# Local attention: one 32x128 matmul for both heads' values of a query tile, and x written by two additions of 64 partitions

## The reference

```python
def _attn_ref(q, k, v):                   # 4 batches, 8 heads, 576 positions, head size 64
    # coarse part: full attention on means of 4 positions (144 x 144), repeated 4 times
    out_up = np.repeat(sm_attn(q_d, k_d, v_d), factor, axis=2)
    # local part: only keys nearer than 4 positions
    mask = np.abs(pos[:, None] - pos[None, :]) < factor
    ... attn = softmax(scale * q @ k^T where mask) ...
    return out_up + attn @ v

a = x @ w1; b = x @ w2                    # first MLP:  2304 x 512 -> 1024
x = ((a * b) @ w3) @ w_out                #             -> 512
h = max(x @ u1, x @ u2, x @ u3)           # second MLP: 512 -> 768
out = h @ u_out                           #             -> 512
```

## Time and profile before

| | before |
|---|---|
| median of 3 runs | 726.11 us (725.23 to 726.60) |
| the profiled execution, its own time | 725.54 us |
| its span, first to last instruction | 723.8 us |
| PE busy | 713.2 us (99%), 6560 matmuls |
| PE weight loads busy | 595.1 us (82%) |
| DVE, ACT, POOL busy | 219.8, 193.0, 210.9 us (30%, 27%, 29%) |
| granted TensorE clock | full in every slice of the span |
| L385 matmuls (local values) | 1536, 18.4 us |
| L571 (x_out) | 16, 12.1 us, 757 ns each |

### The profile page before, as it was taken

One profiled execution on the slowest core, in us unless ns is written; L12 is line 12 of the kernel. 1 busy time (PEld: TensorE's weight loads), 2 busy tenths in 40 slices (PEclk: granted clock), 3 DMA queues, 4 the chain that ended last, 5 costly groups with the idle time before them and its releaser, 6 DMA issues.

```text
span 723.8 us, 14645 instructions
## 1 busy us (share of the span) xinstructions
PE 713.2 (99%) x6560; PEld 595.1 (82%) x6560; DVE 219.8 (30%) x392; ACT 193.0 (27%) x417; POOL 210.9 (29%) x186
## 2 busy tenths in 40 slices
PE   6999999999999999999999999999999999999998
PEld 4778788888888888888888998888888888888898
DVE  3464554414453345411100455111111111111111
ACT  5465423322332233312221533111120112111110
POOL 5799423303232223321220231130122114011210
PEclk9999999999999999999999999999999999999999
DMA  9874122202221121122000320000001000000100
GB/s 321 264 233 142 53 74 74 74 24 75 74 75 54 54 92 58 40 80 81 1 1 0 117 73 1 1 35 24 1 0 60 1 0 25 34 1 1 43 16 29
DMA packets 18590, 43.57 MB, mean 60 GB/s; under 512 B 2144, under 2 KB 2912, under 8 KB 18528
## 3 DMA queue, kind: packets, MB, share of 16 engines
q1 hardware_dynamic: 18528, 42.64, 18.2%
HBM read 37.91 MB, written 4.72 MB: 59 GB/s over the span
## 4 chain that ended last, share of the span: by engine, by line
PE 97%; DMA 1%; POOL 1%; SPq 1%; ACT 0%; DVE 0%; issue 0%
PE psum L346 30%; PE psum L348 29%; PE psum L347 29%; PE psum L385 2%; PE psum L363 2%; PE psum L356 2%; PE psum L394 1%; PE psum L373 1%; DMA attention<-ident 1%; POOL weights_split L738 1%; SPq L310 0%; POOL acts_split L738 0%; ACT attention L622 0%; DVE psum L528 0%; DVE psum L533 0%
## 5 line engine op out<-in xcount | busy, mean ns | idle before, releaser
L346 PE MATMUL psum<-acts_split,weights_split 128*128 128x512 f32 (+1 forms) x992 | 370.3, 373 | 0.6 <-POOL weights_split L738 0.6
L348 PE MATMUL psum<-acts_split,weights_split 128*128 128x512 f32 (+1 forms) x992 | 366.0, 369 | 0.0
L347 PE MATMUL psum<-acts_split,weights_split 128*128 128x512 f32 (+1 forms) x992 | 365.8, 369 | 0.0
L346 PEld LDWEIGHTS psum<-acts_split,weights_split 128*128 128x128 f32 x992 | 187.0, 188 | 34.6 <-issue 2.6
L348 PEld LDWEIGHTS psum<-acts_split,weights_split 128*128 128x128 f32 x992 | 187.0, 189 | 31.7
L347 PEld LDWEIGHTS psum<-acts_split,weights_split 128*128 128x128 f32 x992 | 187.1, 189 | 30.1
L738 POOL TENSOR_TENSOR acts_split<-gate,acts_split 128x512 fp32r<-128x512 f32 (+1 forms) x70 | 82.5, 1179 | 438.0 <-ACT acts_split L622 438.0
L622 ACT ACTIVATE acts_split<-gate 128x512 fp32r<-128x512 f32 (+1 forms) x70 | 41.2, 589 | 246.9 <-DVE gate L608 152.0
L622 ACT ACTIVATE gate<-psum 128x512 f32<-128x512 f32 (+1 forms) x70 | 38.8, 555 | 130.3 <-PE psum L348 130.3
L738 POOL TENSOR_TENSOR acts_split<-xy,acts_split 128x512 fp32r<-128x512 f32 (+1 forms) x44 | 52.2, 1207 | 55.7 <-ACT acts_split L622 55.7
L582 DVE TENSOR_TENSOR gate<-gate,psum 128x512 f32<-128x512 f32 (+1 forms) x40 | 25.4, 634 | 129.0 <-PE psum L348 129.0
(11 more groups left out here) (42 smaller groups left out, 378.4 us busy)
## 6 DMA issues: line engine op xcount, KB each, us to landing
xy<-wa SPq DMA_DIRECT2D x40, 256.0 KB, 5.4
attention<-qk SPq DMA_DIRECT2D x16, 576.0 KB, 4.2
attention<-v_win SPq DMA_DIRECT2D x16, 384.0 KB, 3.4
attention<-wb SPq DMA_DIRECT2D x24, 256.0 KB, 3.0
attention<-v_down SPq DMA_DIRECT2D x16, 320.0 KB, 3.2
out_t<-attention SPq DMA_DIRECT2D x16, 256.0 KB, 2.0
out_t<-attention SPq DMA_DIRECT2D x4, 128.0 KB, 1.7
attention<-mask SPq DMA_DIRECT2D x1, 96.0 KB, 5.7
```

The source lines that it names most:

```text
L346: pe.matmul(out, lhs[:, 0], rhs[:, 0], start=first, stop=False)
L347: pe.matmul(out, lhs[:, 0], rhs[:, 1], start=False, stop=False)
L348: return pe.matmul(out, lhs[:, 1], rhs[:, 0], start=False, stop=last)
```

## The change

Each query tile has one matmul instead of two. The weights are all 128 columns of its 32 key rows (both heads' values), the moving operand is both heads' probabilities side by side (48 columns, in the order head, query). The result is 128 partitions by 48 columns: head 0's values by head 0's probabilities, which are wanted, stand in partitions 0 to 63 of the first 24 columns, and head 1's in partitions 64 to 127 of the last 24. The other two quarters are products of one head's values with the other head's probabilities, and are not read. The place in PSUM grows from 144 to 288 columns of each of the four banks, so it now starts at column 192, and two small sums in bank 4 move from column 400 to 480. Since the wanted columns differ between the two halves of the partitions, `x_out` is now two additions, each of 64 partitions by 576 elements, and only the second signals `x_ready`.

```diff
-        PV = 256
+        PV = TG * TW
...
-        lsum, lsum_eps = (bank(4)[:, 400 + 2 * TG * i:400 + 2 * TG * (i + 1)].rearrange("p (h g) -> p h g", h=2)
+        lsum, lsum_eps = (bank(4)[:, 480 + 2 * TG * i:480 + 2 * TG * (i + 1)].rearrange("p (h g) -> p h g", h=2)
...
-                    for h in range(2):
-                        mm = pe.matmul(bank(4 + i)[D * h:D * (h + 1), PV + TQ * g:PV + TQ * (g + 1)],
-                                       v_sb[rows, g, D * h:D * (h + 1)], prob_t[rows, h, g, own:own + TQ],
-                                       start=True, stop=True)
+                    mm = pe.matmul(bank(4 + i)[:, PV + 2 * TQ * g:PV + 2 * TQ * (g + 1)], v_sb[rows, g, :],
+                                   prob_t[rows, :, g, own:own + TQ], start=True, stop=True)
...
-                local = psum[:, 512 * 4:512 * 8].rearrange("p (i c) -> p i c", i=TI)[:, :, PV:PV + TG * TQ].rearrange(
-                    "p i (g s j) -> p g i s j", g=TG, j=FACTOR)
-                up = up_t.rearrange("p (g i s) -> p g i s", g=TG, i=TI).unsqueeze(4).to_broadcast(
-                    [P, TG, TI, TQ // FACTOR, FACTOR])
+                local = psum[:, 512 * 4:512 * 8].rearrange("p (i c) -> p i c", i=TI)[:, :, PV:PV + 2 * TG * TQ].rearrange(
+                    "p i (g h s j) -> p h g i s j", g=TG, h=2, j=FACTOR)
+                up = up_t.rearrange("p (g i s) -> p g i s", g=TG, i=TI)
...
-                dve.tensor_tensor(out, local, up, ALU.add).then_inc(x_ready, 1)
+                for h in range(2):
+                    rows = slice(D * h, D * (h + 1))
+                    add = dve.tensor_tensor(out[rows], local[rows, h],
+                                            up[rows].unsqueeze(4).to_broadcast([D, TG, TI, TQ // FACTOR, FACTOR]), ALU.add)
+                add.then_inc(x_ready, 1)
```

## The result

The changed kernel takes 732.84 us (median of 4 runs, 732.42 to 733.12) against 725.67 us before (4 runs, 724.99 to 726.60). The ratio is 1.0097, 95% interval 1.0080 to 1.0115: slower by 7.2 us. The profiled execution spans 731.3 us, 7.5 more than before.

The account below looks back on a forecast made before the run. PE was taken as the bound, with L385 limited by instruction count and after the change by array places. Matmuls 6.1, unit 3's S 0.4 and first MLP 0.7 make 7.2 us on 726.11: 733.3 us, range 726.8 to 738.

Parts of the forecast that it names:

- The bound of before: PE's local-value matmuls (L385): instruction count set the 1.08 us per unit, array places at 55 ns a load just below.
- The pace of 8.4 ns from L363: Rate at which PE gets instructions, read from L363's loads; 96 at L385 need 0.81 us, 48 need 0.40.
- The load of 128 columns, 110 ns in its place: L385 on PE: 12 loads of 110 ns in each of four places, +0.38 us a unit, +6.1 us in all.
- The rival in which a load of 128 columns holds its place for 55 ns: L385 on PE: column halves load beside each other, visit stays near 1.08 us, total 727.2; chance 0.07.
- Overlap of load and matmul: L385 on PE: matmuls run beside the next load of their place, so streaming between loads adds no time.
- The rival with both in series: L385 on PE: each load waits for its place's matmul, visit 1.87 us, +12.6 us, total 739.8; chance 0.08.
- The count as the limit: L385 on PE: instructions still decide, 48 fewer save 0.40 us a unit, 6.5 in all, total 720.7; chance 0.12.
- The second addition: x_out on DVE: each half takes a full 758 ns, so x_ready comes 0.68 us later, mostly hidden.
- The overlap of 0.08 us: DVE: two additions with no wait between overlap by 0.08 us, so the second adds 0.68 us, not 0.76.
- Unit 3's S: PE's S visit of unit 3 waits for the later x_out: slack 0.27 us, so +0.4 us, once.
- First MLP: Start of the first MLP: the x_out delay passes through ACT and DVE whole to PE's load, +0.7 us, once.
- Unit 1's S: PE's S visit after unit 0's x_out: slack from the longer V visit, nothing taken, 0.2 us as upper bound.

## Why the prediction was right

The forecast was 733.3 us, measured are 732.84; on the run's own base +7.2 was forecast and +7.2 came. The mechanism is the one that was forecast, but that the numbers meet so closely is luck in part. In the profile the visits, unit 1, unit 3 and the first MLP add up to 8.05 us, 0.85 more than forecast, and some 0.5 us of scatter, most of it in the first 21 us, takes a part of that away. The split between the parts was off too: 6.1 and 1.1 us were forecast for the matmuls and the additions, and alone they cost 5.4 and 2.3.

- **The bound of before** (places at 55 ns a load, and the count above it) holds in its order. With the same 12 loads of 64 columns in a place, 24 matmuls make a visit of 0.84 us and 48 make 1.08. The pace of 8.4 ns from L363 does not fit: 48 loads of local values in eight places need 0.51 us and not 0.40. This pace priced no term of the forecast, since after the change it no longer binds.
- **The load of 128 columns, 110 ns in its place.** Right in size: the fifth load begins some 0.11 us after the first, visit 1.48 for the forecast 1.46. Term: 6.1 forecast, 6.4 in the profile, 5.4 alone by the medians (4.4 to 6.3). The rival in which a load of 128 columns holds its place for 55 ns, so that PE comes out even, is out with it.
- **Overlap of load and matmul** holds: 24 moving columns instead of 48 leave the loads where they are. The rival with both in series had 1.87 us for the changed kernel's visit, which was 1.49, and from there 24 columns would have brought it to 1.24, where it was 1.46. The rule that I weighed against the overlap (the Trainium skill, TensorE: Matmul & The Clock Gate, Part 3, The mechanism: a load overlaps matmuls in flight only on other rows) is not what these runs show.
- **The count as the limit** (the rival on the faster side) falls. Half the count, with the loads in a place as they were, gains 0.24 us (1.08 to 0.84), so it does matter, but doubling the width takes back more than that (0.84 to 1.48). The Trainium skill has some 60 cycles on every matmul (TensorEngine Tiling (Array Packing), Instruction Overhead). By that the prediction had the visit halved to 0.54 us, and it was 1.49.
- **The second addition** costs 755 ns, as 758 for 128 partitions. The overlap of 0.08 us that I took off did not show: two of them take 1.51 and 1.52 us.
- **Unit 3's S**: +0.6 for +0.4. The slack was mis-sized by the missing overlap and by the way from DVE's end to PE's start, 58.93 - 57.26 - 1.52 = 0.15 us here and 0.05 at the program's start.
- **First MLP**: +0.7 as forecast, by the chain that was named.
- **Unit 1's S**: I took nothing, and 0.2 as the bound. It waited 0.48 us, of which 0.35 are left at unit 1's V. The step that failed is "`x_out` starts behind other DVE work that V does not delay": true, but that work waits for a DMA, as the earlier trace rows had it, and it came 0.55 us later than in the profile I had read (22.43 for 21.88), while unit 0's V came 0.45 us earlier (20.41 for 20.86). That this shift belongs to the change is not shown: in the run with 24 columns, with the same two additions, V started at 21.00 and the sums at 22.53, and no wait at unit 1's S is listed.

## What to carry to other kernels

In these runs, small matmuls packed side by side on PE had two limits, and one has to price both: the number of instructions (1.08 us for 48, 0.84 for 24, at the same loads in a place), and for each place in the array the columns of the weights that are loaded into it (0.84 us at 64, 1.48 at 128). Joining two narrow matmuls into one wide one halves the first and, since it also halves the places, doubles the second; join along the rows instead, if zeros in the moving operand are cheap to make (0.98 us here). An addition that was split by partitions cost its full length twice (1.51 us for 0.76), and it is felt where an engine stands at its end, however idle its own engine is.

## What the runs showed of the hardware

- Loads of two tiles on the same rows but in different halves of the columns run beside each other: 24 matmuls in eight places make a visit of 0.68 us, in four 0.84.
- The granted clock fell to 1.2 GHz at the end of or behind seven of sixteen visits of 2.86 us of small matmuls, with PE busy in the profile all the time (3.10 of 3.10 us in the stretch shown). In the profiles with visits of 1.5 us or less it shows no such fall.
- In four places the loads of 128 columns stay 110 ns apart from the first to the last: the 12th in a place begins some 1.2 us after the first, and the 48th of all 1.24 us after.
